# A chunk's attention work on VectorE spread over four projection steps, with values one step later

## The reference

```
def _attn_ref(r, k, v, w, u):              # 2 batches, 8 heads, 768 tokens, 48 channels
    for t in range(S):
        cur = np.einsum('bhd,bhe->bhde', u[None] * kt, vt)
        y[:, :, t] = np.einsum('bhd,bhde->bhe', rt, state + cur)
        state = wt[:, :, :, None] * state + np.einsum('bhd,bhe->bhde', kt, vt)
...
def _moe_ref(x, w_in, w_out):              # 1536 tokens, 384 -> 2048 -> 384
    h = x @ w_in
    g = np.where(h > 0.0, h, alpha * (np.exp(np.minimum(h, 0.0)) - 1.0))
    return (g @ w_out).astype(np.float32)
...
def _moe2_ref(x, domain_probs, w1, w2):    # 4 experts, 384 -> 1024 -> 384
    p = domain_probs / (domain_probs.sum(-1, keepdims=True) + 1e-09)
    for e in range(E):
        out += p[:, e:e + 1] * (np.maximum(x @ w1[e], 0.0) @ w2[e])
```

## Time and profile before

| | us |
|---|---|
| median of 3 runs (lowest, highest) | 741.24 (739.02, 748.74) |
| profiled execution, its own time | 741.96 |
| span of that execution | 740.2 |
| TensorE busy (share of the span) | 703.6 (95%) |
| VectorE, ScalarE, GpSimd busy | 279.9, 180.2, 151.5 |

### The profile page before, as it was taken

One profiled execution on the slowest core, in us unless ns is written; L12 is line 12 of the kernel. 1 busy time (PEld: TensorE's weight loads), 2 busy tenths in 40 slices (PEclk: granted clock), 3 DMA queues, 4 the chain that ended last, 5 costly groups with the idle time before them and its releaser, 6 DMA issues.

```text
span 740.2 us, 10148 instructions
## 1 busy us (share of the span) xinstructions
PE 703.6 (95%) x3966; PEld 624.4 (84%) x3966; DVE 279.9 (38%) x473; ACT 180.2 (24%) x339; POOL 151.5 (20%) x126
## 2 busy tenths in 40 slices
PE   7769988888999999999999999999999999999998
PEld 5659888888787888888898999989999898999987
DVE  7686565565755443332132121313122231212122
ACT  2543232222433344442111111111111111111110
POOL 3843112222201006664000460001630000000000
PEclk9998888888999999999999999999999999999999
DMA  9902222112100003231000220001210000001011
GB/s 338 394 4 76 76 76 76 60 60 61 48 1 1 1 14 94 90 102 44 1 1 0 86 86 1 0 0 43 87 41 1 0 0 1 1 0 43 0 43 44
DMA packets 12854, 38.70 MB, mean 52 GB/s; under 512 B 1552, under 2 KB 3344, under 8 KB 12816
## 3 DMA queue, kind: packets, MB, share of 16 engines
q1 hardware_dynamic: 12528, 37.77, 15.1%
q10 hardware_dynamic: 288, 0.39, 0.1%
HBM read 35.80 MB, written 2.36 MB: 52 GB/s over the span
## 4 chain that ended last, share of the span: by engine, by line
PE 91%; DVE 4%; issue 3%; ACT 1%; DMA 0%; DVEq 0%
PE bank L817 27%; PE bank L819 27%; PE bank L818 27%; PE bank L776 4%; PE bank L772 2%; PE bank L732 1%; PE bank L756 1%; DVE fr L488 1%; PE bank L787 1%; DVE w_lo L573 1%; PE bank L743 1%; DVE fr L496 1%; DVE bank L603 0%; DMA rkw<-rkw_dram 0%; ACT g_hi L428 0%
## 5 line engine op out<-in xcount | busy, mean ns | idle before, releaser
L817 PE MATMUL bank<-x_lo,w_hi 128*128 128x512 f32 (+2 forms) x480 | 185.7, 387 | 6.5 <-DVE g_lo L609 6.0
L674 DVE SCALAR_TENSOR_TENSOR g_lo<-bank,g_hi 128x512 fp32r<-128x512 f32 x96 | 66.4, 692 | 308.4 <-ACT g_hi L457 308.4
L819 PE MATMUL bank<-x_hi,w_hi 128*128 128x512 f32 (+2 forms) x480 | 181.6, 378 | 0.0
L818 PE MATMUL bank<-x_hi,w_lo 128*128 128x512 f32 (+2 forms) x480 | 180.5, 376 | 0.0
L457 ACT ACTIVATE g_hi<-bank 128x512 fp32r<-128x512 f32 x96 | 57.5, 599 | 341.0 <-PE bank L819 341.0
L819 PE MATMUL bank<-w_hi,g_hi 128*128 128x384 f32 x384 | 129.7, 338 | 0.0
L818 PE MATMUL bank<-w_hi,g_lo 128*128 128x384 f32 x384 | 129.6, 337 | 0.0
L817 PE MATMUL bank<-w_lo,g_hi 128*128 128x384 f32 x384 | 129.3, 337 | 0.0
L817 PEld LDWEIGHTS bank<-x_lo,w_hi 128*128 128x128 f32 x480 | 93.1, 194 | 20.7 <-DVE g_lo L609 7.2
L819 PEld LDWEIGHTS bank<-x_hi,w_hi 128*128 128x128 f32 x480 | 93.1, 194 | 17.7
L818 PEld LDWEIGHTS bank<-x_hi,w_lo 128*128 128x128 f32 x480 | 93.4, 194 | 12.8
(11 more groups left out here) (63 smaller groups left out, 595.8 us busy)
## 6 DMA issues: line engine op xcount, KB each, us to landing
raw<-w_dram SPq DMA_DIRECT2D x48, 384.0 KB, 3.1
rkw<-rkw_dram SPq DMA_DIRECT2D x10, 772.5 KB, 4.3
tok<-tok_dram SPq DMA_DIRECT2D x12, 576.0 KB, 4.1
out_dram<-acc SPq DMA_DIRECT2D x10, 192.0 KB, 1.9
rkw<-rkw_dram SPq DMA_DIRECT2D x2, 512.0 KB, 5.0
rkw<-rkw_dram SPq DMA_DIRECT2D x2, 260.5 KB, 4.3
out_dram<-acc ACTq DMA_DIRECT2D x2, 192.0 KB, 2.2
u_rep<-u_dram SPq DMA_DIRECT2D x1, 192.0 KB, 7.4
```

The source lines that it names most:

```text
L674: dve.scalar_tensor_tensor(out=g2[1][:, r, :], in0=p_h[j % 2][:, :], scalar=0.0, in1=g2[0][:, r, :].bitcast(F32), op0=ALU.max, op1=ALU.sub ...
L817: pe.matmul(out, wh, ml, start=start, stop=False)
L818: pe.matmul(out, wl, mh, start=False, stop=False)
L819: return pe.matmul(out, wh, mh, start=False, stop=stop)
```

## The change

In VectorE's steps the pieces of a chunk's attention move to other steps, counted from the step s of its scores:

| piece | before | after |
|---|---|---|
| `products` of the chunk | s-5, after lo_g | s-3, after lo_g |
| `inverses` | s-4 | s-2 |
| `scale_k` | s-3 | s-2 |
| `scale_r` | s-2 | s-1 |
| `scale_state` | s, after lo_g | s-1, between elu and lo_g |
| `bonus` | s, after lo_g | s, between elu and lo_g |
| `mask_scores` | s+1, both halves before elu | s+1, one half before elu, one after |
| `finish_y` | s+2, before elu | s+3, before elu |
| `add_update`, `lo_x` | s+3 | s+4, before elu |

On TensorE `values` goes from s+1 to s+2, `update` and `turn_y` from s+2 to s+3; `hi_x` on ScalarE from s+3 to s+4, ahead of the activations. GpSimd works in pieces of 192 columns instead of 384 in `bonus_terms` and `lo_w`; slices 11 and 13 go from VectorE to GpSimd, slice 0 the other way, slice 9 is split after step 3 instead of 4, and VectorE's splits come in two halves of 384 columns. In the prologue four `warm` matmuls go, `update(1)` comes after both `turn_y`, GpSimd takes r.u.k of chunk 1 and VectorE only the u product of chunk 0, `bonus(0)` comes ahead of the mask of chunk 1.

```diff
-LO_VECTOR = (3, 5, 7, 9, 11, 13)
-LO_POOL = (0, 1, 2, 4, 6, 8, 10, 12, 14, 15)
-LO_AFTER = {0: 3, 1: 5, 2: 7, 4: 9, 6: 11, 8: 13}
+LO_VECTOR = (0, 3, 5, 7, 9)
+LO_POOL = (1, 2, 4, 6, 8, 10, 11, 12, 13, 14, 15)
+LO_AFTER = {0: 3, 1: 5, 2: 7, 3: 9}
+PIECES = 4
...
@@ gpsimd @@
-                r, k = tok[c % DEEP][:, 0:DM], tok[c % DEEP][:, DM:2 * DM]
-                pool.tensor_tensor(r, r, k, ALU.mult).then_inc(s_rk, 1)
-                pool.wait_ge(s_rk, c * 2 + 1)
-                pool.tensor_tensor(r, r, u_rep[:, :], ALU.mult).then_inc(s_rk, 1)
+                t = tok[c % DEEP]
+                for r, k in zip(column_halves(0), column_halves(DM)):
+                    pool.tensor_tensor(t[:, r], t[:, r], t[:, k], ALU.mult).then_inc(s_rk, 1)
+                for i, r in enumerate(column_halves(0)):
+                    pool.wait_ge(s_rk, rk_done(c - 1) + i + 1)
+                    pool.tensor_tensor(t[:, r], t[:, r], u_rep[:, r], ALU.mult).then_inc(s_rk, 1)
...
@@ vector, steps @@
                 for c in due(n, 1):
-                    mask_scores(c, BESIDE)
-                for c in due(n, 2):
+                    mask_scores(c, 0, BESIDE)
+                for c in due(n, 3):
                     finish_y(c, BESIDE)
+                for c in due(n, 4):
+                    if c < NUPDATE:
+                        add_update(c, BESIDE)
+                    lo_x(c, BESIDE["yt"])
                 elu(n)
-                for c in due(n, 3):
-                    lo_x(c, BESIDE["yt"])
+                for c in due(n, 0):
+                    bonus(c)
+                for c in due(n, 1):
+                    mask_scores(c, 1, BESIDE)
+                for c in due(n, -1):
+                    scale_state(c)
+                if n in LO_AFTER:
+                    lo_w(LO_AFTER[n], 0)
...
                 if n in LO_AFTER:
-                    lo_w(LO_AFTER[n])
-                for c in due(n, 0):
-                    bonus(c)
-                    scale_state(c)
-                for c in due(n, -5):
+                    lo_w(LO_AFTER[n], 1)
+                for c in due(n, -3):
                     products(c)
-                for c in due(n, -4):
+                for c in due(n, -2):
                     inverses(c)
-                for c in due(n, -3):
                     scale_k(c)
-                for c in due(n, -2):
+                for c in due(n, -1):
                     scale_r(c)
...
@@ tensor, prologue and steps @@
             update(0, BANKS0)
-            warm(1, 2)
             values(1, BANKS1)
+            turn_y(0, BANKS0)
+            turn_y(1, BANKS1)
             update(1, BANKS1)
-            turn_y(0, BANKS0)
-            warm(1, 1)
-            turn_y(1, BANKS1)
-            warm(1, 1)
...
-                for c in due(n, 1):
+                for c in due(n, 2):
                     values(c, BESIDE)
-                for c in due(n, 2):
+                for c in due(n, 3):
                     if c < NUPDATE:
                         update(c, BESIDE)
                     turn_y(c, BESIDE)
```

More of the change, by code:

```diff
@@ L158, in bass_linear_attention_elu_ffn_dense_experts @@
         s_rk = sem("s_rk")
+        s_ru = sem("s_ru")
         s_bon = sem("s_bon")
@@ L216, in slice_ready @@
             if n in LO_VECTOR:
-                eng.wait_ge(s_wv, LO_VECTOR.index(n) + 1)
+                eng.wait_ge(s_wv, LO_VECTOR.index(n) * 2 + 2)
             else:
-                eng.wait_ge(s_wq, LO_POOL.index(n) * 2 + 2)
+                eng.wait_ge(s_wq, LO_POOL.index(n) * PIECES + PIECES)
         def slot_of(e, j):
@@ L240, in due, with rk_done, column_halves @@
             return [c for c, step in SCORES.items() if step + offset == n]
+        def rk_done(c):
+            return 3 + 4 * (c - 1)
+        def column_halves(first):
+            return slice(first, first + DM // 2), slice(first + DM // 2, first + DM)
         def width(n):
@@ L346, in lo_w @@
                 pool.wait_ge(s_wh, n + 1)
-                for half in (slice(0, DM), slice(DM, 2 * DM)):
-                    pool.tensor_tensor(w_lo[:, n, half], raw[:, n, half], w_hi[:, n, half].bitcast(F32),
+                for i in range(PIECES):
+                    part = slice(i * (2 * DM // PIECES), (i + 1) * (2 * DM // PIECES))
+                    pool.tensor_tensor(w_lo[:, n, part], raw[:, n, part], w_hi[:, n, part].bitcast(F32),
                                        ALU.subtract).then_inc(s_wq, 1)
@@ L362, in _ @@
             pool.tensor_tensor(tok[0][:, 0:DM], tok[0][:, 0:DM], tok[0][:, DM:2 * DM], ALU.mult).then_inc(s_rk, 1)
-            pool.wait_ge(s_rk, 2 * FIRST)
-            lo_w(0)
+            pool.wait_ge(s_qp, FIRST)
+            landed(pool, s_tok, 1)
+            pool.tensor_tensor(tok[1][:, 0:DM], tok[1][:, 0:DM], tok[1][:, DM:2 * DM], ALU.mult).then_inc(s_rk, 1)
+            pool.wait_ge(s_u, 16)
+            pool.wait_ge(s_rk, 2)
+            pool.tensor_tensor(tok[1][:, 0:DM], tok[1][:, 0:DM], u_rep[:, :], ALU.mult).then_inc(s_rk, 1)
             bonus_v(0)
@@ L372, in _ @@
             lo_w(8)
+            lo_w(10)
+            lo_w(11)
             bonus_terms(3)
-            lo_w(10)
             bonus_v(2)
             lo_w(12)
+            lo_w(13)
             lo_w(14)
@@ L437, in _ @@
             for n in range(STEP1):
+                for c in due(n, 4):
+                    hi_x(c, BESIDE["yt"])
                 exponential(n)
@@ L441, in _ @@
                         copy_kt(c, BESIDE)
-                for c in due(n, 3):
-                    hi_x(c, BESIDE["yt"])
                 if n % J1 == LAG - 1 and n > LAG:
@@ L520, in scale_r, with mask_scores @@
                                   ALU.mult).then_inc(s_qp, 1)
[L522 to L527, removed]
+            def mask_scores(c, o, banks):
+                if o == 0:
+                    dve.wait_ge(s_px, c + 1)
+                    need(dve, s_py, c)
+                dve.tensor_tensor(att[:, o, :, :], banks["x"][o][:, :].rearrange("p (a t) -> p a t", a=PAIRS),
+                                  mask.unsqueeze(1).broadcast_to([P, PAIRS, CH]), ALU.mult).then_inc(s_att, 1)
             def add_update(c, banks):
@@ L543, in bonus @@
             def bonus(c):
-                dve.wait_ge(s_rk, c * 2 + 2)
+                if c == 0:
+                    dve.wait_ge(s_ru, 1)
+                else:
+                    dve.wait_ge(s_rk, rk_done(c))
                 need(dve, s_cv, c - 1)
@@ L548, in bonus @@
                                   AX.X, ALU.add).then_inc(s_bon, 1)
[L550 to L554, removed]
             def finish_y(c, banks):
@@ L568, in lo_x, with lo_w @@
                                   x_hi[:, :, chunk(c)].bitcast(F32), ALU.subtract).then_inc(s_x, 1)
-            def lo_w(n):
+            def lo_w(n, half):
                 dve.wait_ge(s_wh, n + 1)
-                dve.tensor_tensor(w_lo[:, n, :], raw[:, n, :], w_hi[:, n, :].bitcast(F32),
+                part = slice(half * DM, (half + 1) * DM)
+                dve.tensor_tensor(w_lo[:, n, part], raw[:, n, part], w_hi[:, n, part].bitcast(F32),
                                   ALU.subtract).then_inc(s_wv, 1)
@@ L581, in _ @@
             dve.wait_ge(s_const, 16)
-            mask_scores(0, BANKS0)
+            mask_scores(0, 0, BANKS0)
+            mask_scores(0, 1, BANKS0)
             inverses(1)
@@ L586, in _ @@
             dve.wait_ge(s_u, 16)
[L587 to L591, removed]
+            dve.wait_ge(s_rk, 1)
+            dve.tensor_tensor(tok[0][:, 0:DM], tok[0][:, 0:DM], u_rep[:, :], ALU.mult).then_inc(s_ru, 1)
             bonus(0)
+            mask_scores(1, 0, BANKS1)
+            mask_scores(1, 1, BANKS1)
             bonus(1)
+            lo_w(0, 0)
+            lo_w(0, 1)
             finish_y(0, BANKS0)
@@ L646, in _ @@
                     lo_x2(n // J1 - 1, 2)
-                for c in due(n, 3):
-                    if c < NUPDATE:
-                        add_update(c, BESIDE)
                 if n == 0:
@@ L782, in turn_y @@
                 pe.wait_ge(s_y, 2 * c + 2)
+                pe.wait_ge(s_kt, min(c + 1, NUPDATE))
                 if banks is BESIDE:
-                    pe.wait_ge(s_kt, min(c + 1, NUPDATE))
                     pe.wait_ge(s_x, c)
```

## The result

The changed kernel takes 700.02 us (median of 4 runs, 696.13 to 701.63) against 744.99 us for the kernel before on the same chip (4 runs, 739.02 to 748.78). The ratio is 0.940, with a 95% interval of 0.931 to 0.948. The profiled execution took 701.63 us, with a span of 699.6 us against 740.2.

A forecast was written before the change was run, and what follows sets the result against it. TensorE waiting for VectorE's late mask, with the low clock, was taken to bound the narrow tiles. Gains 28 + 5.2 + 0.6 + 7.8 + 2.6 + 1.5 - 1.7 = 44.0 us off 741.96 gave 698 us, range 691 to 715.

The forecast's parts named there:

- The bound and its price: Narrow-tile periods: TensorE waits 2.87 us for VectorE's mask, the low clock loses 3.5 us; 14.25 us needed instead of 20.36.
- The new order against a TensorE that never waits: Narrow-tile schedule with each VectorE piece's due time; finish_y has 0.4 us in hand; five periods gain 28 us together.
- 1.0 us for step 17: Deduction in the narrow tiles: three lo_x2 pieces stand ahead of finish_y at step 17, costing 1.0 us.
- hand-overs: Deduction in the five narrow-tile periods: 0.3 us a period for hand-overs, 1.5 us together.
- Contention leaves the steady part: Narrow tiles: scans come when GpSimd waits, both near 1.24 us, alpha near 0.2 us.
- steps 0 to 7: Stretch 23.4 to 46.1 us: half splits in VectorE's holes gain 2.6 us; removed warming costs 1.7 us.
- Chunk 2 to 3: First chunk beside the projections, 23.0 us before: 14.25 us needed plus 1 us of hold-ups, gain 7.8 us.
- Prologue: Start to first up projection: removing warming matmuls and reordering gain 1.5 us, 0.3 to 2.5.
- Rival 2: The clock still falls once a chunk, after values' long run of 48-column matmuls; 722 us, chance 0.1.
- rival 1: finish_y becomes the late piece, delaying update and turn_y by 1.5 us in each of eight periods; 710 us, chance 0.2.
- rival 3: Slower: late finish_y makes elu, scale_r and scores slide, TensorE idles longer at low clock; up to 765 us, chance 0.03.
- rival 4: The mask is not what values waited for, so nothing much moves; 738 us, chance 0.03.

The follow-up runs named there:

- one-half kernels: x_values and x_spread, each the kernel with one half of the change; 705.84 and 703.2 us.
- x_values: Kernel before with values, update and turn_y one step later, finish_y, lo_x, add_update and hi_x with them; VectorE's scans, bonus and state scaling unmoved; 705.84 us.
- yardstick: The changed kernel run again unedited on another chip, giving its second profile; 701.5 us (696.24 to 704.07).
- third profile: Profile of the changed kernel, unedited, run again on the chip of the 96-column and filling kernels; 698.51 us, ratio 0.940.
- x_spread: Changed kernel with values, update and turn_y back in their old steps, both mask halves ahead of elu, finish_y, lo_x and add_update one step earlier; 703.2 us.

## Why the prediction was right

**The bound and its price** (2.87 us of gap, 3.5 us of low clock, 14.25 us needed): right. Four of five periods measured 14.26 to 14.28 us, and both one-half kernels lose the gap, x_values with the old scan, alpha and mask still in their old order. One reading was loose: rows 5 show the r.k product beside the scan, but what held up the scan was the y product of chunk 4 ahead of it:

```profile
91.89 0.88 POOL L339 TENSOR_TENSOR y_sb<-tok,bonus_sb 128x384 f32<-128x384 f32 x1 [16.52 <-DVE bonus_sb L547]
```

It ends at 92.77 us, and the scan 1.09 us later. The r.k product in turn ends after the scan, and alpha after the r.k product.

**The new order against a TensorE that never waits**: right in each of its times to about 0.5 us. finish_y had 0.8 us in hand where I gave it 0.4. The 1.0 us for step 17 was wrong: that period took 14.26 us. The hand-overs cost nothing measurable, where I took 1.5 us. The other way, one of the five periods was 15.8 us, since the clock fell in it. The sum, 29.0 against 28, is right because these errors cancel.

**Contention leaves the steady part**: right, 1.23 and 0.14 us. That smaller pieces bound a hold-up, as I took from the Trainium skill, page "SBUF — State Buffer", section on the two separate sides (the first to start has the shared ports "for the whole instruction"), does not hold: in the stretch up to chunk 3 a VectorE instruction was passed over by up to about eighteen GpSimd instructions. The measurement decides. The profile that was taken first has none above 1.63 us, so this did not enter its numbers. In the yardstick's profile, with its 4.50 us, steps 0 to 7 take 27.0 us instead of 22.3.

**Chunk 2 to 3**, 7.1 us where I had 7.8: near by luck. The 1.0 us of hold-ups in my sum cost nothing, since TensorE is busy for 15.87 of the 15.90 us, and what is above 14.25 us is a fall of the clock (0.89) that I did not have there. In the third profile, without that fall, the stretch takes 14.3 us.

**Prologue, 1.5 us**: wrong in that profile (-0.1), and the sign that I gave for it, a first up projection later than 22.5 us, came (23.53). The step that failed is the clock: I held the low stretch to 3.4 us, and it was (1 - 0.78) x 2 x 23.5 = 10.3 us within the prologue. The reordering itself is worth some 3 us at that clock (23.53 and 23.22 us against 26.56 and 26.54). I also blamed the removed warming for a low stretch, and no run bears that out: the two profiles at 26.5 us have the warming and the same low stretch. In two later profiles of the same code the first up projection starts at 21.1 and 21.2 us. Steps 0 to 7 gained 0.4 us instead of 2.6 - 1.7 = 0.9. GpSimd's slices 10 and 12 were ready at 42.4 and 50.9 us, some 3 us later than I put them, and no up projection waited for them. The scores of chunk 3, forecast for 57 to 59 us, start at 61.7 us in the first profile and at 57.4 us in the third.

**Rival 2, the clock falls whatever stands ahead**: half right, and I gave its counter-evidence too much weight. Two of the ten chunks from 2 on show it with TensorE busy without a break, and so do two in the second profile of this kernel and one in the third. The first:

```profile
67.60:70.60 3.00, 3.00 (x34) 2.95 (x34) 2.49 (x7) 0.37 (x1) 0.00 (x0) 1.00 0.02 5
70.60:74.20 3.60, 3.60 (x20) 3.38 (x21) 2.10 (x7) 1.17 (x3) 0.00 (x0) 0.55 0.63 211
```

The first row is values of chunk 3 (48-column matmuls) at clock 1.00, the second what follows, at 0.55. Chunk 10's values are followed by the same, which is the -0.5 us of the wide tiles.

**Rivals 1, 3 and 4** did not come. The 2.2 us of hold-up that rival 1 names is not in its rows: the scan's 1.87 against 1.23 us and alpha's 0.88 against 0.14 us make 1.4 us. x_spread shows what one late piece costs, though it is another one, scale_r ahead of scores: 0.5 us a period. It also shows step 17's pieces costing 0.65 us more where no time is in hand.

## What to carry to other kernels

Find what stands ahead of the awaited instruction in its own engine's queue, then either move that behind it or move the consumer one step on; either was worth some 40 us here, both together little more. Lay the new order out against a bounding engine that never waits, with each piece's due time: it gave the periods without a fall of the clock to 0.1 us. Do not cut a GpSimd job into pieces issued back to back in order to let VectorE in; leave a wait between them, or leave them whole. In time only the 96-column pieces were clearly worse here; 192 and 384 columns can't be told apart. Compare two versions of a prologue only at the same granted clock.

## What was not expected of the hardware

One VectorE instruction (here a subtraction or a scan) can be held up by a whole unbroken run of GpSimd instructions: 4.50, 4.09, 4.08 and 6.22 us with 192-column splits, 7.34 and 7.43 us with 96 columns, none above 2.1 us with 384 columns (in five profiles) or with a wait between 96-column pieces (one profile). It does not happen each time; why it does in one run and not in the next stays open.

The granted clock can fall after 3.0 us of 48-column matmuls without any idle time: in three profiles of the changed kernel it does so behind 5 of 30 chunks, 0.3 to 0.4 us after values ends, for 3.4 us. Every other fall in its steps comes during, or within 2 us of, idle time of TensorE. Up to the first up projection the same code has a mean clock of 0.78 in the first profile and 0.93 in the third, some 10 and 3 us at 1.2 GHz. Over the sixteen runs of that code time and mean clock go together, so such differences are most of the spread between 696 and 704 us. What sets when the clock falls was not tried.
